# One block with a single test per engine, and the last tile stored in four blocks

## The reference

```
scale = min(|a|, 0.999) / (|a| + 1e-6);  ar, ai = a_re*scale, a_im*scale
S_re, S_im = ar*S_re - ai*S_im + k v^T,  ar*S_im + ai*S_re      # per time step
y[t] = q[t] @ S_re
```

## Time and profile before

| what | us |
|---|---|
| median of 3 runs | 1082.45 (1082.26 to 1083.61) |
| profiled execution, its own time | 1079.82 |
| its span, first to last instruction | 1078.0 |
| PE busy | 1026.5 (95%) |
| DVE busy | 697.0 (65%) |
| ACT busy | 597.8 (55%) |

### The profile page before, as it was taken

One profiled execution on the slowest core, in us unless ns is written; L12 is line 12 of the kernel. 1 busy time (PEld: TensorE's weight loads), 2 busy tenths in 40 slices (PEclk: granted clock), 3 DMA queues, 4 the chain that ended last, 5 costly groups with the idle time before them and its releaser, 6 DMA issues.

```text
span 1078.0 us, 18324 instructions
## 1 busy us (share of the span) xinstructions
PE 1026.5 (95%) x7014; PEld 919.0 (85%) x7014; DVE 697.0 (65%) x1382; ACT 597.8 (55%) x1151; POOL 2.8 (0%) x17
## 2 busy tenths in 40 slices
PE   1779999999999999999999999999999999999995
PEld 1668899998888888888888899999999999998995
DVE  5899998887777777887753366545445454454442
ACT  7888888877667777776452266423333233332321
POOL 1000000000000000000000000000000000000000
PEclk9989999999999999999999999999999999999998
DMA  6554432323223222321010053101010010100000
GB/s 111 122 120 105 80 67 42 56 54 58 38 38 67 37 38 39 84 42 23 2 37 2 2 175 127 42 1 59 1 43 18 1 59 1 54 6 1 30 1 32
DMA packets 176013, 51.57 MB, mean 48 GB/s; under 512 B 151472, under 2 KB 172080, under 8 KB 175920
## 3 DMA queue, kind: packets, MB, share of 16 engines
q1 hardware_dynamic: 175920, 50.35, 21.5%
HBM read 40.89 MB, written 9.44 MB: 47 GB/s over the span
## 4 chain that ended last, share of the span: by engine, by line
PE 88%; DVE 6%; ACT 3%; issue 1%; DMA 0%; POOL 0%; SPq 0%; DVEq 0%; POOLq 0%; ACTq 0%
PE ph L702 36%; PE acc L720 31%; PE even L720 5%; PE odd L808 2%; PE even L776 2%; PE odd L776 2%; PE even L768 2%; PE odd L768 2%; PE chain L728 1%; PE even L787 1%; PE chain L752 1%; PE even L796 1%; PE chain L735 1%; PE even L791 1%; PE even L800 1%
## 5 line engine op out<-in xcount | busy, mean ns | idle before, releaser
L702 PE MATMUL ph<-x_hi,win_hi 128*128 128x512 f32 (+2 forms) x624 | 239.6, 384 | 1.6 <-DVE x_lo L603 1.6
L473 DVE TENSOR_TENSOR g_lo<-gf,g_hi 128x512 fp32r<-128x512 f32 (+2 forms) x208 | 134.6, 647 | 164.5 <-ACT g_hi L303 164.4
L702 PE MATMUL ph<-x_hi,win_lo 128*128 128x512 f32 (+2 forms) x624 | 235.3, 377 | 0.0
L702 PE MATMUL ph<-x_lo,win_hi 128*128 128x512 f32 (+2 forms) x624 | 234.7, 376 | 0.0
L303 ACT CAST g_hi<-gf 128x512 fp32r<-128x512 f32 (+2 forms) x208 | 122.0, 586 | 170.5 <-PE even L720 128.7
L295 ACT ACTIVATE gx<-ph 128x512 f32<-128x512 f32 (+2 forms) x208 | 117.4, 565 | 141.7 <-PE ph L702 141.5
L702 PEld LDWEIGHTS ph<-x_hi,win_hi 128*128 128x128 f32 x624 | 117.7, 189 | 21.2 <-issue 4.5
L702 PEld LDWEIGHTS ph<-x_hi,win_lo 128*128 128x128 f32 x624 | 117.4, 188 | 19.8
L702 PEld LDWEIGHTS ph<-x_lo,win_hi 128*128 128x128 f32 x624 | 117.6, 188 | 15.5
L720 PE MATMUL acc<-g_hi,wout_hi 128*128 128x512 f32 (+2 forms) x336 | 126.5, 377 | 0.7 <-DVE g_lo L473 0.7
L720 PE MATMUL acc<-g_hi,wout_lo 128*128 128x512 f32 (+2 forms) x336 | 121.1, 360 | 0.0
(11 more groups left out here) (130 smaller groups left out, 1604.4 us busy)
## 6 DMA issues: line engine op xcount, KB each, us to landing
wraw<-in_moe_w_out SPq DMA_DIRECT2D x32, 192.0 KB
gate<-in_a_re SPq DMA_DIRECT2D x24, 192.0 KB, 3.1
gate<-in_a_im SPq DMA_DIRECT2D x24, 192.0 KB, 3.5
qk<-in_q SPq DMA_DIRECT2D x24, 192.0 KB, 3.1
qk<-in_k SPq DMA_DIRECT2D x24, 192.0 KB, 3.8
rot<-hidden SPq DMA_DIRECT2D x6, 768.0 KB, 5.8
out<-res SPq DMA_DIRECT2D x6, 768.0 KB, 4.3
vs<-in_v SPq DMA_DIRECT2D x24, 128.0 KB, 4.1
```

The source lines that it names most:

```text
L473: vec.tensor_tensor(gs[1][:, n % 2, 0:size], gf[:, n % 2, 0:size], gs[0][:, n % 2, 0:size].bitcast(F32), ALU.subtract).then_inc(g_lo, 1)
L702: ins = mm(ph[n % 2][:, 0:size], win[hi][:, j, kc], xs[lo][:, T % 2, kc, 0:size], start=i == 0, stop=i == KC * len(PARTS) - 1)
```

## The change

The two general blocks are no blocks any more. `attention_any` and `mlps_any` return functions, one per engine, and `fused` calls them at the end of each engine's stream under a single test. All waits and bodies of the general path stay as they are. The test waits for `judged`, which `verdict` now raises when it has written the word. On SP the test stands behind the issue of the last stores and ahead of the wait for their landing. The last tile has functions of its own: `down` raises `last_made` behind each of the first three blocks of its last item; ACT copies block 0 and, after `f_used`, block 3; DVE copies blocks 1 and 2; and SP issues four DMAs of 128 rows, each when its block has been copied.

```diff
-def fused(nc, q, k, v, a_re, a_im, weights, out, hidden, weak):
+def fused(nc, sem, q, k, v, a_re, a_im, weights, out, hidden, weak, attention, mlps):
...
+        def is_weak(eng):
+            eng.wait_ge(judged, 1)
+            return eng.value_load(weak[0:1, 0:1], min_val=0, max_val=1) > 0
...
+            def store_last():
+                tok = tiles[-1][1]
+                for m, (copied, count) in enumerate(((last_act, 1), (last_dve, 1), (last_dve, 2), (last_act, 2))):
+                    sp.wait_ge(copied, count)
+                    sp.dma_start(out[tok + m * P:tok + (m + 1) * P, :], res[:, m * E:(m + 1) * E]).then_inc(stored, 16)
...
-            sp.wait_ge(stored, 16 * len(tiles))
+            with sp.If(is_weak(sp)):
+                sp.wait_ge(stored, 16 * (len(tiles) - 1 + TB))
+                sp.sem_inc(restart, 1)
+                attention[0](sp)
+                sp.sem_inc(x_there, 1)
+                mlps[0](sp)
+            sp.wait_ge(stored, 16 * (len(tiles) - 1 + TB))
...
+            def last_result():
+                act.wait_ge(stored, 16 * (len(tiles) - 1))
+                act.wait_ge(last_made, 1)
+                sc.copy(res[:, 0:E], accs[0][:, 0:E]).then_inc(last_act, 1)
+                act.wait_ge(f_used, ITEMS)
+                sc.copy(res[:, 3 * E:4 * E], accs[3][:, 0:E]).then_inc(last_act, 1)
...
+            with act.If(is_weak(act)):
+                act.wait_ge(restart, 1)
+                attention[1](act)
+                act.wait_ge(x_there, 1)
+                mlps[1](act)
...
+            def last_result():
+                dve.wait_ge(stored, 16 * (len(tiles) - 1))
+                for m in (1, 2):
+                    dve.wait_ge(last_made, m + 1)
+                    vec.tensor_copy(res[:, m * E:(m + 1) * E], accs[m][:, 0:E]).then_inc(last_dve, 1)
...
-                step(vec.tensor_scalar(weak[:], flags[:], 0.5, None, ALU.is_lt))
+                vec.tensor_scalar(weak[:], flags[:], 0.5, None, ALU.is_lt).then_inc(judged, 1)
...
+            with dve.If(is_weak(dve)):
+                dve.wait_ge(restart, 1)
+                attention[2](dve)
+                dve.wait_ge(x_there, 1)
+                mlps[2](dve)
...
+                    if n == ITEMS - 1 and m < TB - 1:
+                        ins.then_inc(last_made, 1)
                 ins.then_inc(f_used, 1)
...
+            with pe.If(is_weak(pe)):
+                pe.wait_ge(x_there, 1)
+                mlps[3](pe)
```

More of the change, by code:

```diff
@@ L144, in fused @@
         stored = sem("stored")
+        last_made, last_act, last_dve = sem("last_made"), sem("last_act"), sem("last_dve")
+        judged, restart, x_there = sem("judged"), sem("restart"), sem("x_there")
         block = ctx.enter_context(nc.Block())
+        def is_weak(eng):
+            eng.wait_ge(judged, 1)
+            return eng.value_load(weak[0:1, 0:1], min_val=0, max_val=1) > 0
         def weight_at(a):
@@ L258, in _ @@
                         store_hidden(T)
+                    elif T < len(tiles) - 1:
+                        store_out(T)
                     else:
-                        store_out(T)
+                        store_last()
                 if (x := x_step_at(a + 2)) is not None and x[1] == 0:
@@ L408, in _ @@
                 if (T := finished_at(a)) is not None:
-                    result(T)
+                    if T < len(tiles) - 1:
+                        result(T)
+                    else:
+                        last_result()
                 if (x := x_step_at(a)) is not None:
@@ L876, in attention_any, with on_sp @@
         LOADS = 5 * H
[L877 to L892, removed]
+        def on_sp(sp):
+            sp.sem_inc(y_ready, 1)
+            sp.sem_inc(y_stored, 16)
+            with sp.Fori(0, B) as b:
+                with sp.Fori(0, CN) as c:
+                    n = b * CN + c
+                    sp.wait_ge(y_ready, n + 1)
+                    for dst, src in ((ar, a_re), (ai, a_im), (qs, q), (ks, k)):
@@ L898, in _ @@
[L898 to L909, removed]
@@ L911, in _ @@
-        @block.vector
-        def _(dve):
+                    for h in range(H):
+                        sp.dma_start(vs[h * R:(h + 1) * R],
+                                     v[b, h, bass.ds(c * TC, TC), :].rearrange("t (r e) -> r t e", e=ER)) \
+                            .then_inc(loaded, 16)
+                    sp.wait_ge(y_ready, n + 2)
+                    sp.dma_start(scratch[:, bass.ds(n * TC, TC)].rearrange("(p e) t -> p e t", e=ER), y[:]) \
+                        .then_inc(y_stored, 16)
@@ L913, in _, with on_act, on_dve @@
+            sp.wait_ge(y_stored, (B * CN + 1) * 16)
+            sp.dma_start(X[:, :, :], scratch.rearrange("(c p) t -> p c t", p=P)).then_inc(x_back, 16)
+            sp.wait_ge(x_back, 16)
+        def on_act(act):
+            with act.Fori(0, B * CN) as n:
+                act.wait_ge(m2_ready, n + 1)
+                nc.scalar.activation(mag[:], m2[:], ACT.Sqrt).then_inc(mag_ready, 1)
+        def on_dve(dve):
             vec = nc.vector
             NORM, STEP = 7, 8
[L915 to L965, removed]
-                                                      qs[:, bass.ds(i, 1), :].broadcast_to([P, ER, D]), ALU.mult), 7)
-                            vec.tensor_reduce(y[:, :, bass.ds(i, 1)].rearrange("p e t -> p (e t)"), kv[:],
-                                              mybir.AxisListType.X, ALU.add).then_inc(step_chain, 1)
-                        dve.wait_ge(step_chain, (n * TC + TC) * STEP + 1)
-                        dve.sem_inc(y_ready, 1)
@@ L975, in mlps_any @@
+    return on_sp, on_act, on_dve
+def mlps_any(nc, sem_any, weights, X, out):
     N, D = out.shape
@@ L1124, in tile, with on_dve @@
                         split_x(*nxt, 1 - r, j - XSTEP)
-            with act.If(act.value_load(weak[0:1, 0:1], min_val=0, max_val=1) > 0):
-                for kc in range(KC):
-                    split_x(0, 0, 0, 0, kc)
-                for j in range(WS):
-                    split_w(0, j)
-                tiles(act, tile)
-                split_g(2 * TILES - 1, FC - 1)
-                result(1, 2 * TILES - 1, (TILES - 1) * TOK)
-        @block.vector
-        def _(dve):
+            for kc in range(KC):
+                split_x(0, 0, 0, 0, kc)
+            for j in range(WS):
+                split_w(0, j)
+            tiles(act, tile)
+            split_g(2 * TILES - 1, FC - 1)
+            result(1, 2 * TILES - 1, (TILES - 1) * TOK)
+        def on_dve(dve):
             vec = nc.vector
@@ L1193, in tile, with on_pe @@
                         split_x(*nxt, 1 - r, j - XSTEP)
-            with dve.If(dve.value_load(weak[0:1, 0:1], min_val=0, max_val=1) > 0):
-                for kc in range(KC):
-                    split_x(0, 0, 0, 0, kc)
-                for j in range(WS):
-                    split_w(0, j)
-                tiles(dve, tile)
-                split_g(2 * TILES - 1, FC - 1)
-                result(1, 2 * TILES - 1, (TILES - 1) * TOK)
-        @block.tensor
-        def _(pe):
+            for kc in range(KC):
+                split_x(0, 0, 0, 0, kc)
+            for j in range(WS):
+                split_w(0, j)
+            tiles(dve, tile)
+            split_g(2 * TILES - 1, FC - 1)
+            result(1, 2 * TILES - 1, (TILES - 1) * TOK)
+        def on_pe(pe):
             PARTS = ((0, 0), (0, 1), (1, 0))
@@ L1244, in tile @@
                     down(layer, T, j)
-            with pe.If(pe.value_load(weak[0:1, 0:1], min_val=0, max_val=1) > 0):
-                for j in range(AHEAD):
-                    up(0, 0, 0, j)
-                tiles(pe, tile)
+            for j in range(AHEAD):
+                up(0, 0, 0, j)
+            tiles(pe, tile)
+    return on_sp, on_act, on_dve, on_pe
 def program(nc, q, k, v, a_re, a_im, moe_w_in, moe_w_out, moe2_w_in, moe2_w_out, out):
@@ L1256, in program, with sem @@
     weights = ((moe_w_in, moe_w_out), (moe2_w_in, moe2_w_out))
-    with nc.sbuf_tensor("weak", [1, 1], mybir.dt.int32) as weak:
-        fused(nc, q, k, v, a_re, a_im, weights, out, hidden, weak)
+    with ExitStack() as ctx:
+        def sem(name):
+            return ctx.enter_context(nc.semaphore(name))
+        weak = ctx.enter_context(nc.sbuf_tensor("weak", [1, 1], mybir.dt.int32))
         with nc.sbuf_tensor("X", [P, H * D // P, B * S], F32) as X:
-            attention_any(nc, q, k, v, a_re, a_im, X, weak, scratch)
-            mlps_any(nc, weights, X, out, weak)
+            attention = attention_any(nc, sem, q, k, v, a_re, a_im, X, scratch)
+            mlps = mlps_any(nc, sem, weights, X, out)
+        fused(nc, sem, q, k, v, a_re, a_im, weights, out, hidden, weak, attention, mlps)
 _INS = ["q", "k", "v", "a_re", "a_im", "moe_w_in", "moe_w_out", "moe2_w_in", "moe2_w_out"]
```

106 lines of the change are left out of this document (72 added, 34 removed).

## The result

The changed kernel takes 1075.77 us (median of 4 runs, 1075.17 to 1076.48) where the kernel before takes 1082.36 (4 runs): ratio 0.9938, 95% interval 0.9921 to 0.9955, so 6.6 us less by the medians, 4.9 to 8.6 by the interval. Forecast were 1075.4 us.

The account below looks back on a forecast made before the run. Bound: PE, busy 1026.5 of 1078.0 us, with 11.5 us behind its last matmul. Of these 4.5 remain, so 7.0 us less: 1082.45 to 1075.4 us, range 1073.9 to 1078.3; 94% for faster.

Parts of the forecast that it names:

- The split of the 11.5 us: Behind the last matmul: copies 1.1, store 3.6, first block's barrier 0.3, first test 1.8, second test 4.7 us, in a row.
- Part 1, copies and stores: Last tile: copies and stores by block bring the store's landing to 1068.9 us from 1071.2, 2.3 us earlier.
- SP keeps up: SP's first three store issues, 0.5 us apart at 0.38 us each, are through at 1067.46 us.
- Part 2, tests under cover: Program end: two of three barriers go; engines test and fetch code beside other work and the store; last engine at 1070.5 us.
- the allowance for the store: Program end: 0.2 us added because code fetches run next to store packets; bounds 0 and 1 us.
- early reading: Word load does not wait for matmuls or copies: PE through at 1068.3, ACT at 1070.1, DVE at 1070.0 us.
- drain and barrier: 0.3 us: Program end: 0.3 us from PE's branch end to the release, taken from the last block of before.
- A: Program end: the last of ACT, DVE and PE behind its code fetch ends the program; 1075.4 us, 50%.
- B: Program end: SP's joint jump misses too and SP is last; gain 6.4 us, 1076.0 us; 30% together with another rival.
- C: Program end: poor overlap, fetches get through only after the store lands or partly in turn; gain 5.1 us, 1077.3 us; 14%.
- D: Program end: fetches do not overlap, stalls follow one another; slower by 2.6 us, 1085.0 us, 2%; half as no change, 4%.
- a branch over 4 us: Sign at the program end: branch gaps over 4 us would show C or D.

Follow-up runs that it names:

- four_stores_three_blocks: The kernel before with only the last tile's copies and four stores changed, its three blocks and seven tests kept: 1079.67 us, ratio 0.9984.
- two_stores: The changed kernel with PE's code shifted by four instructions and the last tile stored in two DMAs of 256 rows: 1074.97 us, ratio 0.9938.
- pe_code_shifted_again: Repeat of the changed kernel with four more PE instructions at its start (waits long true): 1075.19 us, ratio 0.9937.
- after_again: The changed kernel run once more, nothing changed: 1075.15 us, ratio 0.9935.

## Why the prediction was right, and where it was not

The gain came from where the prediction has it, the two blocks that fall away and the tests that move under work. Two of its terms failed, and an error in the last step of the sum covered for them.

- **The split of the 11.5 us** was right, and with it the reading of the stalls as code loads behind far branches. Without the general path the tail is 3.0 us, and 2.8 by the pieces.
- **Part 1, copies and stores.** Copies on time. Fourth issue forecast at 1067.1, measured at 1069.1; landing forecast at 1068.9, measured at 1071.3. The step that failed is "SP keeps up": it rests on an issue of 0.38 us and holds only with no code packet near (`four_stores_three_blocks`: landing at 2.6 us of tail, where the forecast is 2.4); two of the issues took 1.9 and 1.1 us. I had allowed 0.2 us, at most 1, for fetches beside the store, and only on the side of the fetches; the store paid 2.4 us.
- **Part 2, tests under cover.** Right that each engine tests and loads while the rest works: PE's test began at 1063.7 (forecast 1063.9), and the last of PE, ACT and DVE drained at 1070.2 (forecast 1070.5, or 1070.7 with the allowance for the store). Right too, in its early reading, that the word load waits for no copy: ACT's starts with its last copy. PE's branch was put at 3.4 us and took 5.3; it began early enough to hide this.
- **Last on the way out.** The step "drain and barrier: 0.3 us" failed by 1.9 us in the one profile and 0.8 in the other; the traces point to a further code packet for which PE waits there. The step took the barrier of before as the measure, but its cost hangs on where PE's code lies.
- **Which engine ends it.** Neither A nor B as told. In A the last of ACT, DVE and PE ends the program; it was SP's landing, 1.1 us behind them, and then PE's release. B's missed jump did not come: SP's joint hop takes at most 0.9 us (1070.4 to 1071.3, and in this time the landing was due as well). The Trainium skill speaks in "Runtime: NRT & Kernel Launch", section "Instruction fetch mechanics", of a fetch for a target outside the two blocks held, and by its blocks of 16 KiB the joint hop, estimated at 200 instructions and more, stays inside. The trace agrees: a miss cost 2.7 to 2.9 us on ACT and DVE before. That the packets are of 8 KB did not make it miss.
- **C and D.** Fetches and store did hinder each other, which is C in kind: its tail would have been 6.4 us, between the two of the changed kernel. Its sign, a branch over 4 us, came too (5.3 in the first profile). D, one stall after another, is refuted: the three drains lie within 0.2 us in the first profile and 2.2 in the second.
- **The number.** The profiled time was forecast at 1072.8 and was 1075.2, so 2.4 us off; by the second profile (1073.68) 0.9. That the median was met to 0.4 us is luck in the sum's last step: I took the 2.6 us between timed and profiled runs of before over to the changed kernel, where it was 0.6, and these 2.0 us cancel most of the 2.4. The profiled run of before was one of its fastest.
- **By its own signs.** The prediction calls itself wrong if the span does not end between 1069.5 and 1073. The first profile ended at 1073.6, outside; the second at 1072.1, inside.

## What to carry to other kernels

A test that skips a long body cost a code load of 2.5 to 5.3 us on each of PE, ACT and DVE here, so it belongs where the engine still has work in flight or others do; with four stores, the seven tests in blocks of their own cost this kernel 7.1 us of tail (10.1 against 3.0), and one per engine under cover 1.7 (4.7 against 3.0, PE's code shifted). Code packets hold up the stores beside them, in their issue and in their landing: whoever puts the one under the other must add the store's delay to the sum. And the tail of a change like this one can gain or lose 1 to 2 us by where the code of one engine happens to lie; shift it by a few instructions before believing such a difference.

## What the runs showed that I had not expected

PE's branch over the same body took 3.4 to 5.3 us, in two profiles of one kernel 5.3 and 3.4. These two differ in PE's packets from 1065 to 1067.9 us: two of 16 KB beside each other in the first (1.5 and 2.0 us long), one in the second (0.95 us). Why there are two stays open.

```profile
q8 instruction: 2, 0.03, 7.6%
q8 instruction: 1, 0.02, 2.0%
```

And the place of the last matmul moves between runs, at 1066.3 to 1070.7 us, by something that is over by about 92 us: from the first matmul of the fifth item (88.1 us in before, 92.3 in `two_stores`) to the end of the last matmul it is 978.4 us in both. The granted clock in the stretch from 50 to 70 us is 0.83 in the profile of before and 0.58 in that of `two_stores`, and from 70 to 92 it is 0.92 against 0.84. Rows of the windows view, first before, then `two_stores` (the last three numbers: granted clock, DMA share, GB/s):

```profile
50.00:70.00 20.00, 13.68 (x142) 12.19 (x143) 19.43 (x44) 16.07 (x33) 0.00 (x0) 0.83 0.57 131
70.00:92.00 22.00, 19.41 (x207) 18.57 (x207) 20.18 (x45) 19.82 (x45) 0.00 (x0) 0.92 0.54 116
```

```profile
50.00:70.00 20.00, 15.35 (x128) 13.82 (x128) 17.52 (x39) 15.48 (x30) 0.00 (x0) 0.58 0.56 129
70.00:92.00 22.00, 18.71 (x190) 17.61 (x186) 18.22 (x42) 16.84 (x36) 0.00 (x0) 0.84 0.39 89
```

A low clock from 50 to 70 us does not fix it: `pe_code_shifted_again` had 0.57 there and 1.00 from 70 to 92, and its last matmul ended at 1066.5. I had put these stretches before 35 us in the expectation of `after_again`, which was wrong. This is the scatter in which the medians above drown differences of 1 us, and why tails were compared.
